# Attention with a token mix behind it: when GpSimd starts a pair's work, which output ScalarE drains first, and VectorE's order in the third step

## The chip, the cores and the metric

The kernel runs on one core of a Trainium2 chip. A core has five engines that run in parallel, each in its own program order: TensorE (PE in the profile; its weight loads are PEld), VectorE (DVE), ScalarE (ACT), GpSimd (POOL), and SyncE (SP), which issues the transfers. They wait for one another through counting semaphores. The metric is the device time of one execution in microseconds (us).

## The reference

Three layers in float32. The change touches the first and the hand-over to the second.

```python
# attention: 4 batches x 8 heads, 576 tokens, 64 channels per head
scores = 0.125 * q @ k.T
scores = where(scores >= max(scores) - tau, scores, -1e9)
attn = exp(scores - max(scores)); attn /= attn.sum() + 1e-9
x = attn @ v                                   # heads side by side: 576 x 512 per batch
# layer 2: token mix, then channel mix
u = x + (relu(x.T @ w_tok1) @ w_tok2).T         # 576 -> 256 -> 576 tokens
u = u + relu(u @ w_ch1) @ w_ch2                 # 512 -> 1536 -> 512
# layer 3: gated convolution over tokens
h = relu(u @ w_in); out = (h * sigmoid(conv3(h))) @ w_out
```

## The kernel before

**Units and steps.** Two heads make a pair; there are 16 pairs. The 576 queries of a pair are cut into five units: t = 0 to 3 hold 128 queries of both heads, t = 4 holds the last 64 queries of both. The function `bodies` calls a `body` on each engine for k = 0 to 18: k counts the pairs, and k = 16 to 18 only finish the last ones. `at.g` is the pair's number, `at.k` the same number as far as it is known when the program is built (k = 4 to 13 run in a hardware loop of two pairs, an even one and an odd one, for five turns). On PE, DVE and ACT a body has five steps s = 0 to 4.

**Softmax of a unit.** PE makes its scores (`scores`, L999, L1004). DVE copies them negated out of PSUM and takes the maximum (`copy_out`, L841). ACT makes exponentials and threshold (`exp_unit`, L591, L594). DVE masks (`mask`, L858): it reads the negated scores and the exponentials, both in SBUF, and writes `prob`. PE turns `prob` (L1025, L1034; the 64 columns that are left over are turned by L1064 and L1079 and called tails), and ACT drains what was turned into `probT` (`drain_turned_probs`, L608, L615, L617) and `probTt` (L624, L625, L631). In step s of pair g PE makes the scores of unit s+2 and turns those of unit s, and DVE copies unit s+2 and masks unit s+1, where s+2 and s+1 run over into the next pair.

**The output of a pair.** The product of pair g-1 with its values (PV) is made in steps 0 and 1 of body g: `times_v` (L1094), then `times_v_tail` (L1102), which raises `pv_done`. In step 2 ACT drains it to `oT` (L641 to L644), PE turns it (L1120, and L1112 in step 3), and the rows are scaled into `x32`: the last 64 queries by ACT in step 2 (`normalise_short`, L662, raises `short_x`), the other 512 by DVE in step 3 (`normalise`, L881, raises `x_done`). PE turns `x32` back in step 4 (`turn_back`, L1125, raises `xt_done`), and ACT drains that into `uy` (`drain_x`, L667, raises `xt_drained`).

There is one `x32`. Both who write it wait until the pair before has been split by GpSimd; `pair` is g-1 here, and `x_split` counts the pairs that are split:

```python
# ScalarE, normalise_short(pair, k), step 2
act.wait_ge(xa_tail_done, pair + 1)
act.wait_ge(inv_done, pair + 1)
if k >= 1:
    act.wait_ge(x_split, pair)
# VectorE, normalise(pair, k), step 3
if k >= 1:
    dve.wait_ge(x_split, pair)
```

TensorE's tail in step 3 (`turn_tails(at, 3)`, L1079 into `mixed`) waits for `short_x` of the same step.

**GpSimd's work.** Products in the mixes take each operand as a rounded part and a rest. GpSimd makes these: `split_x` (xh, L440, then the rest xl, L471), `rest_of_token` (h1l, L490, twice for two pairs together), the weights (`split_wt`, `split_weight`, `split_w1`), and `add_u` adds a pair's token mix to `uy` (L498). PE makes the token mix for two pairs at a time: in odd bodies `mix_hidden` (L1146, steps 3 and 4; waits for `x_split`), in even bodies `mix_out` (L1175: half a pair's output in step 2, the other half in step 3, and the next pair's in step 4; the first piece waits for `tok_lo`, which `rest_of_token` raises). ACT drains these in `drain_hidden` (L650, L651) and `drain_u` (L673). The first tails of each pair (`turn_first_tails`, L1064, end of step 0) go into the banks `mixed` and `out_t` and wait for these drains (`wait_for_banks`): for `hid_left` in even bodies, for `u_drained` in odd ones.

Of the kernel before, what the change touches and what calls it, by code (L numbers as in the profile page):

```python
# [22 lines left out]
P = 128  # L23

def build(nc, qk_in, v_in, tau, w_tok1, w_tok2, w_ch1, w_ch2, w_in, conv_w, w_out, out):
    PAIRS, _, S = qk_in.shape
# [16 lines left out]
    KM, KF, KC, KT = DM // P, DF // P, DC // P, DT // P  # L44
# [150 lines left out]
    with ctx:  # L195
# [38 lines left out]
        pv_done = sem("pv_done")  # L234
# [195 lines left out]
        def _(pool):  # L430
# [27 lines left out]
            xs_hi = sem("xs_hi")  # L458

            def split_x(at):  # L460
                pair = at.g - 1
                mine = slice((at.k - 1) % 2 * P, (at.k - 1) % 2 * P + P)
                pool.wait_ge(x_done, pair + 1)
                pool.wait_ge(short_x, pair + 1)
                if at.hid:
                    pool.wait_ge(tok_done, at.g - 1)
                pool.nop(nofuse=True)
                copy(xh[:, :, mine], x32[:, :, :]).then_inc(xs_hi, 1)
                pool.wait_ge(xs_hi, pair + 1)
                pool.nop(nofuse=True)  # L470
                nc.gpsimd.tensor_tensor(xl[:, :, mine], x32[:, :, :], xh[:, :, mine].bitcast(F32), ALU.subtract) \  # L471
                    .then_inc(x_split, 1)
# [12 lines left out]

            def rest_of_token(at, i):

                pool.wait_ge(hid_left, at.g - 2 + i)
                pool.nop(nofuse=True)
                nc.gpsimd.tensor_tensor(h1l[:, i, :], h1f[:, i, :], h1h[:, i, :].bitcast(F32), ALU.subtract) \  # L490
                    .then_inc(tok_lo, 1)
# [24 lines left out]

            def body(at):
                g, k = at.g, at.k
                if at.mix:
                    add_u(g - 4)  # L520
                for i in range(KT if at.hid else 0):
                    rest_of_token(at, i)
                if at.pv:
                    split_x(at)
                if at.mix:
                    add_u(g - 3)
                if k == 1:
                    split_wt(range(NT))
                if k == 2:
                    for kt in range(KT):  # L530
                        split_weight(wt2h[:, kt, :], wt2l[:, kt, :], wt2f[:, kt, :], wt_split)
                if k % 2 == 1 and k < 2 * W1_EARLY:
                    split_w1(g // 2, k == 1)

            bodies(pool, body)

            for c in range(W1_EARLY, KC):
                split_w1(c, False)
# [38 lines left out]
        def _(act):  # L577
# [124 lines left out]
            def body(at):  # L702
                g, k = at.g, at.k
                for s in range(NT):
                    if s == 0 and k == PAIRS:
                        round_first_u(0)
                        round_first_u(1)
                    if s == 2 and at.pv:
                        drain_out(g - 1, k - 1)
                    if s == 2 and at.units:  # L710
                        drain_first_tails(at)
                    if at.units:
                        drain_turned_probs(at, s)
                    if s == 4 and at.pv:
                        act.wait_ge(xt_done, g)
                        if not at.units:
                            drain_x_tail(g - 1)
                        drain_x(g - 1)
                    ahead = at.unit(s + 2)
                    if ahead:  # L720
                        exp_unit(ahead)
                    if s == 2:
                        if at.mix:
                            drain_u(g - 4, 0, 0)
                        if at.pv:
                            normalise_short(g - 1, k - 1)
                        if at.units:
                            drain_tail(at, 2)
                        if k == PAIRS + 1:
                            unit(0, 2, 3)  # L730
                    if s == 3:
                        if at.hid:
                            drain_hidden(at, 0)
                        if at.mix:
                            drain_u(g - 4, 1, 1)
                        if at.units:
                            drain_tail(at, 3)
                        if PAIRS <= k < PAIRS + 2:
                            unit(0, 3 * (k - PAIRS), 3 * (k - PAIRS) + 1)
                    if s == 4:  # L740
                        if at.hid:
                            drain_hidden(at, 1)
                        if at.mix:
                            drain_u(g - 3, 0, 1)
                            drain_u(g - 3, 1, 0)
                        if k == PAIRS:
                            unit(0, 1, 2)
# [74 lines left out]
        def _(dve):  # L822
# [76 lines left out]
            def body(at):  # L899
                for s in range(NT):  # L900
                    two, one = at.unit(s + 2), at.unit(s + 1)
                    if two:
                        copy_out(two)
                    if s == 4 and at.units:
                        invert_sums(at)
                    if one:
                        mask(one)
                    if s == 1 and at.k == PAIRS:
                        split_first_u()
# [463 lines left out]
```

## Time and profile before

| | |
|---|---|
| median of 3 runs | 849.05 us (848.79 to 851.71) |
| the profiled execution's own time | 850.66 us |
| its span in the trace | 848.9 us |
| busy share of the span: PE, PEld, DVE, ACT, POOL | 97%, 79%, 50%, 49%, 31% |
| granted TensorE clock, mean | 0.997 of full speed |
| chain of work that ended last: PE, DVE, ACT, issue | 84%, 6%, 6%, 3% |

The span is the time from the first to the last instruction of the trace; some 1.8 us of the execution lie around it. The shares are means over the three layers. The pairs fill the first 320 us or so, layer 2's channel mix the time to about 643 us, the third layer the rest. From k = 4 on the pairs repeat every 40.1 us for an even and an odd one together. A mean over the span says little of that stage, so the rows below are of two pairs in the middle of it, the even pair from about 168 us and the odd one from about 188 us.

### The profile page before, as it was taken

How to read it: one execution, taken by the hardware profiler on the slowest of the kernel's cores; microseconds unless marked ns; L12 is line 12 of the kernel's file. 1: busy time of each engine (PE TensorE's matmuls, PEld its weight loads, DVE VectorE, ACT ScalarE, POOL GpSimd, SP SyncE). 2: the span in 40 equal slices, each digit the busy share in tenths (PEclk: the TensorE clock that was granted, in tenths of full speed). 3: DMA queues.
4: the chain of work that ended last, by engine and by line, in shares of the span. 5: the costliest groups of instructions: out<-in, count | busy, mean ns of one | idle time of the engine just before them, and what ended most of it. 6: DMA issues, size and time to landing. Idle time of an engine off the chain costs nothing.

```text
span 848.9 us, 15131 instructions
## 1 busy us (share of the span) xinstructions
PE 824.3 (97%) x5656; PEld 669.5 (79%) x5656; DVE 422.5 (50%) x829; ACT 412.5 (49%) x914; POOL 265.7 (31%) x202
## 2 busy tenths in 40 slices
PE   8999999999999998899999999999999999999998
PEld 4666776767777766788888888888899989898996
DVE  6897878787877774501211211211214819156380
ACT  4887887877878785211211201211114737355461
POOL 0062415142332323470200100120291726428170
PEclk9999999999999999999999999999999999999999
DMA  9311111111111114000000000000320010100101
GB/s 266 111 48 47 48 48 46 46 46 46 46 46 46 50 16 149 1 1 0 1 1 1 0 1 1 1 0 1 128 71 2 1 51 1 45 17 0 49 0 62
DMA packets 20906, 32.70 MB, mean 39 GB/s; under 512 B 4416, under 2 KB 11136, under 8 KB 20864
## 3 DMA queue, kind: packets, MB, share of 16 engines
q1 hardware_dynamic: 20864, 32.13, 11.7%
q8 instruction: 28, 0.46, 0.2%
q14 instruction: 14, 0.11, 0.0%
HBM read 27.41 MB, written 4.72 MB: 38 GB/s over the span
## 4 chain that ended last, share of the span: by engine, by line
PE 84%; DVE 6%; ACT 6%; issue 3%; POOL 0%; ACTq 0%; DVEq 0%; POOLq 0%
PE score L1203 17%; PE score L1318 12%; PE score L999 5%; PE out_t L1218 4%; PE turn_y L1218 4%; PE mixed L1218 4%; PE turn_x L1218 4%; DVE prob L858 4%; PE out_t L1303 4%; PE out_t L1094 4%; PE mixed L1146 3%; PE mixed L1094 3%; PE turn_y L1303 3%; PE mixed L1303 3%; PE turn_x L1303 3%
## 5 line engine op out<-in xcount | busy, mean ns | idle before, releaser
L921 DVE SCALAR_TENSOR_TENSOR h<-score,h 128x512 fp32r<-128x512 f32 (+1 forms) x60 | 38.3, 638 | 243.5 <-ACT h L693 243.5
L693 ACT ACTIVATE h<-score 128x512 fp32r<-128x512 f32 (+1 forms) x60 | 33.3, 555 | 250.5 <-PE score L1203 250.5
L841 DVE TENSOR_SCALAR_CACHE_REDUCE negs<-score,neg_scale 128x576 f32<-128x576 f32 x144 | 112.7, 816 | 58.7 <-PE score L999 34.0
L858 DVE SCALAR_TENSOR_TENSOR prob<-negs,thresh,exps 128x576 f32<-128x576 f32 x144 | 134.2, 964 | 0.3 <-ACT thresh L594 0.3
L591 ACT ACTIVATE exps<-negs,neg_max 128x576 f32<-128x576 f32 x144 | 104.6, 772 | 1.9 <-DVE negs L841 1.5
L999 PE MATMUL score<-qk 64*128 64x288 f32 x512 | 85.5, 434 | 1.6 <-DVE negs L841 1.0
L1203 PE MATMUL score<-uh,w1h 128*128 128x512 f32 (+1 forms) x240 | 86.9, 368 | 0.0
L1203 PE MATMUL score<-uh,w1l 128*128 128x512 f32 (+1 forms) x240 | 86.8, 368 | 0.0
L1203 PE MATMUL score<-ul,w1h 128*128 128x512 f32 (+1 forms) x240 | 86.8, 368 | 0.0
L559 POOL TENSOR_TENSOR zl<-z,zh 128x512 fp32r<-128x512 f32 x32 | 54.2, 1694 | 98.7 <-ACT zh_t L779 98.7
L999 PEld LDWEIGHTS score<-qk 64*128 64x128 f32 x512 | 46.9, 188 | 28.0 <-issue 13.1
L506 POOL TENSOR_TENSOR ul<-uy,uh 128x256 fp32r<-128x256 f32 (+6 forms) x7 | 16.7, 2402 | 161.7 <-ACT uh L680 161.7
L961 DVE SCALAR_TENSOR_TENSOR conv<-hpad,cw,conv 128x576 f32<-128x576 f32 x32 | 27.2, 850 | 77.4 <-ACT conv L792 77.3
L1025 PEld LDWEIGHTS turn_x<-ident,prob 64*128 64x128 f32 x512 | 41.4, 139 | 22.1 <-issue 16.4
L608 ACT ACTIVATE probT<-turn_x 128x512 f32<-128x512 f32 x64 | 38.2, 596 | 41.0 <-PE turn_y L1025 40.3
L1318 PE MATMUL score<-yl,wih 128*128 128x288 f32 x256 | 54.9, 296 | 0.0
L1318 PE MATMUL score<-yh,wil 128*128 128x288 f32 x256 | 54.8, 296 | 0.0
L1318 PE MATMUL score<-yh,wih 128*128 128x288 f32 x256 | 54.8, 296 | 0.0
L1025 PE MATMUL turn_x<-ident,prob 64*128 64x64 f32 x512 | 46.8, 225 | 6.4 <-DVE prob L858 4.3
L490 POOL TENSOR_TENSOR h1l<-h1f,h1h 128x256 fp32r<-128x256 f32 x16 | 11.7, 728 | 127.7 <-ACT h1f L651 127.7
L1203 PEld LDWEIGHTS score<-uh,w1l 128*128 128x128 f32 x240 | 45.3, 189 | 7.6
L1203 PEld LDWEIGHTS score<-ul,w1h 128*128 128x128 f32 x240 | 45.3, 189 | 7.6
(184 smaller groups left out, 2010.0 us busy)
## 6 DMA issues: line engine op xcount, KB each, us to landing
qk<-in_qk SPq DMA_DIRECT2D x16, 640.0 KB, 3.9
vm<-in_v SPq DMA_DIRECT2D x16, 320.0 KB, 4.2
result<-ostage SPq DMA_DIRECT2D x16, 256.0 KB, 2.1
w1f<-in_moe_w_ch SPq DMA_DIRECT2D x4, 768.0 KB, 10.8
w2f<-in_moe_w_ch SPq DMA_DIRECT2D x4, 768.0 KB, 7.4
wif<-in_moe_w_in SPq DMA_DIRECT2D x1, 2048.0 KB, 7.8
wof<-in_moe_w_out SPq DMA_DIRECT2D x8, 256.0 KB, 2.6
wt2f<-in_moe_w_tok SPq DMA_DIRECT2D x1, 576.0 KB, 9.4
```

The source lines that it names most:

```text
L559: nc.gpsimd.tensor_tensor(zl[:, t, :], z32[:, t % 2, 0:MAIN], zh[:, t, :].bitcast(F32), ALU.subtract)
L591: nc.scalar.activation(exps[i][:, h, :], negs[:, i, h, :], ACT.Exp, bias=neg_max[:, i, h:h + 1], scale=-1.0).then_inc(exp_done, 1)
L841: nc.vector.tensor_scalar(negs[:, i, h, :].rearrange("p (c s) -> p c s", c=2), raw_of[h], neg_scale[:, 0:1], None, ALU.mult, ALU.min, accu ...
L858: nc.vector.scalar_tensor_tensor(out=prob[:, i, h * S:(h + 1) * S], in0=negs[:, i, h, :], scalar=thresh[:, i, h:h + 1], in1=exps[i][:, h, ...
L921: nc.vector.scalar_tensor_tensor(out=h3[:, n % RING, 1, 0:w], in0=hidden_banks[n % 4][:, 0:w], scalar=0.0, in1=h3[:, n % RING, 0, 0:w].bit ...
L999: mm = nc.tensor.matmul(score[:, 2 * h + c, 0:HALF], qT[par][rows, t * P:(t + 1) * P], kT[par][rows, halves[c]])
L1025: mm = nc.tensor.transpose(turn[r][:, to:to + D], prob[rows, i, k_at:k_at + P], ident[rows, rows])
L1094: nc.tensor.matmul(bank[mine, 0:HALF], vm[par][:, kt, mine], probT[par][:, h, kt, c * HALF:(c + 1) * HALF], start=(kt == 0), stop=False, s ...
L1203: mm = nc.tensor.matmul(hidden_banks[n % 4][:, 0:w], wt[:, c, kt, :], x[:, kt, 0:w], start=(i == 0), stop=(i == 3 * KM - 1))
L1218: mm = nc.tensor.matmul(sum_banks[mt][:, 0:w], wt[:, c, o:o + P], h3[:, n % RING, part, 0:w], start=(c == 0 and i == 0), stop=(c == KC - 1 ...
L1303: mm = nc.tensor.matmul(bank, z, wt[:, kt, :], start=(kt == 0 and n == 0), stop=(kt == KF - 1 and n == 2))
L1318: mm = nc.tensor.matmul(in_banks[c % 2][:, i, 0:HALF], wt[:, kt, c * P:(c + 1) * P], y[:, kt, i * HALF:(i + 1) * HALF], start=(n == 0), st ...
```

## The change

Three edits. On GpSimd each body that has a PV waits for it first. The parts of its work move by a body: the split of a pair's `x32` and the rest of the hidden tokens are made one body later than before, and the two `add_u` stand elsewhere. On ScalarE the drain of the output turned back (`drain_x`) stands ahead of the drain of the turned probabilities in step 4. On VectorE the mask of unit 3 stands ahead of the copy of unit 4 in step 2, the third step.

```diff
             def split_x(at):
-                pair = at.g - 1
-                mine = slice((at.k - 1) % 2 * P, (at.k - 1) % 2 * P + P)
+                pair = at.g - 2
+                mine = slice(at.k % 2 * P, at.k % 2 * P + P)
                 pool.wait_ge(x_done, pair + 1)
                 pool.wait_ge(short_x, pair + 1)
-                if at.hid:
-                    pool.wait_ge(tok_done, at.g - 1)
+                if at.mix:
+                    pool.wait_ge(tok_done, at.g - 2)
+                if 5 <= at.k and at.k % 2 == 1:
+                    pool.wait_ge(tok_done, at.g - 3)
                 pool.nop(nofuse=True)
...
             def rest_of_token(at, i):
 
-                pool.wait_ge(hid_left, at.g - 2 + i)
+                pool.wait_ge(hid_left, at.g - 3 + i)
...
             def body(at):
                 g, k = at.g, at.k
-                if at.mix:
+                if at.pv:
+                    pool.wait_ge(pv_done, g)
+                for i in range(KT if at.mix else 0):
+                    rest_of_token(at, i)
+                if k >= 5 and k % 2 == 1:
                     add_u(g - 4)
-                for i in range(KT if at.hid else 0):
-                    rest_of_token(at, i)
-                if at.pv:
+                if 2 <= k < PAIRS + 2:
                     split_x(at)
-                if at.mix:
-                    add_u(g - 3)
...
                 if k % 2 == 1 and k < 2 * W1_EARLY:
                     split_w1(g // 2, k == 1)
+                if at.mix:
+                    add_u(g - 4)
 
             bodies(pool, body)
+            add_u(PAIRS - 1)
...
                     if s == 2 and at.units:
                         drain_first_tails(at)
-                    if at.units:
-                        drain_turned_probs(at, s)
                     if s == 4 and at.pv:
                         act.wait_ge(xt_done, g)
                         if not at.units:
                             drain_x_tail(g - 1)
                         drain_x(g - 1)
+                    if at.units:
+                        drain_turned_probs(at, s)
...
             def body(at):
                 for s in range(NT):
                     two, one = at.unit(s + 2), at.unit(s + 1)
+                    if one and s == 2:
+                        mask(one)
                     if two:
                         copy_out(two)
                     if s == 4 and at.units:
                         invert_sums(at)
-                    if one:
+                    if one and s != 2:
                         mask(one)
```

**GpSimd, one turn of the hardware loop.** This is the even body and then the odd one, before. In the names x is `x32`, h1l and h1f are the hidden tokens' rest and value.

```order
L498 TENSOR_TENSOR uy<-u_part,uy 128x576
L440 TENSOR_SCALAR xh<-x_81 128x5x128 [waits x_done,short_x]
L471 TENSOR_TENSOR xl<-x_81,xh 128x5x128 [waits xs_hi]
...
L498 TENSOR_TENSOR uy<-u_part,uy 128x576
...
L490 TENSOR_TENSOR h1l<-h1f,h1h 128x256 [waits hid_left] x2
...
L440 TENSOR_SCALAR xh<-x_81 128x5x128 [waits tok_done,x_done,short_x]
L471 TENSOR_TENSOR xl<-x_81,xh 128x5x128 [waits xs_hi]
...
L447 TENSOR_TENSOR w1h<-w1f,ones 128x512
...
L483 TENSOR_TENSOR w1l<-w1f,w1h 128x512 [waits chunk_hi]
```

And the same turn of the changed kernel:

```order
L490 REGISTER_ALU [waits pv_done]
L492 TENSOR_TENSOR h1l<-h1f,h1h 128x256 [waits hid_left]
...
L492 TENSOR_TENSOR h1l<-h1f,h1h 128x256 [waits hid_left]
...
L440 TENSOR_SCALAR xh<-x_81 128x5x128 [waits tok_done,x_done,short_x]
L473 TENSOR_TENSOR xl<-x_81,xh 128x5x128 [waits xs_hi]
...
L500 TENSOR_TENSOR uy<-u_part,uy 128x576
...
L496 ISA [waits pv_done]
...
L500 TENSOR_TENSOR uy<-u_part,uy 128x576
L440 TENSOR_SCALAR xh<-x_81 128x5x128 [waits tok_done,x_done,short_x]
L473 TENSOR_TENSOR xl<-x_81,xh 128x5x128 [waits xs_hi]
```

The even body now begins behind `pv_done` with both h1l, then xh and xl, then one addition; the odd body behind its `pv_done` with an addition, then xh and xl, then the weights as before. The xh and xl of an even body belonged to the pair whose PV that body finished; now they belong to the pair ahead of it.

**VectorE, steps 1 to 3 of an even pair in the loop.** L841 is a copy, L858 a mask, L881 `normalise`. Before:

```order
L858 SCALAR_TENSOR_TENSOR prob,rowsum<-negs,thresh,exps_71 128x576
...
L858 SCALAR_TENSOR_TENSOR prob,rowsum<-negs,thresh,exps_71 128x576
...
L841 TENSOR_SCALAR negs,neg_max<-score,neg_scale 128x576
...
L858 SCALAR_TENSOR_TENSOR prob,rowsum<-negs,thresh,exps_79 128x576
...
L858 SCALAR_TENSOR_TENSOR prob,rowsum<-negs,thresh,exps_79 128x576
...
L841 TENSOR_SCALAR negs,neg_max<-score,neg_scale 128x576 x2
```

And of the changed kernel:

```order
L863 SCALAR_TENSOR_TENSOR prob,rowsum<-negs,thresh,exps_71 128x576
...
L863 SCALAR_TENSOR_TENSOR prob,rowsum<-negs,thresh,exps_71 128x576
...
L863 SCALAR_TENSOR_TENSOR prob,rowsum<-negs,thresh,exps_79 128x576
...
L863 SCALAR_TENSOR_TENSOR prob,rowsum<-negs,thresh,exps_79 128x576
...
L846 TENSOR_SCALAR negs,neg_max<-score,neg_scale 128x576
...
L846 TENSOR_SCALAR negs,neg_max<-score,neg_scale 128x576 x2
```

The two masks of unit 3 (exps_79) now follow straight on those of unit 2, and the single copy of unit 4 comes behind them.

**ScalarE, step 4 of an even pair in the loop**, before:

```order
L631 ACTIVATE probTt_72<-mixed 128x128
...
L599 ACTIVATE uy<-turn_x 128x64
L615 ACTIVATE probT_74<-turn_x 128x4x64
L617 ACTIVATE probTt_72<-turn_x 64x64
L615 ACTIVATE probT_74<-turn_y 128x4x64
L617 ACTIVATE probTt_72<-turn_y 64x64
...
L667 ACTIVATE uy<-out_t 128x512
...
L591 ACTIVATE exps_71<-negs,neg_max 128x576
```

And of the changed kernel:

```order
L636 ACTIVATE probTt_72<-mixed 128x128
...
L672 ACTIVATE uy<-out_t 128x512
...
L604 ACTIVATE uy<-turn_x 128x64
L620 ACTIVATE probT_74<-turn_x 128x4x64
L622 ACTIVATE probTt_72<-turn_x 64x64
L620 ACTIVATE probT_74<-turn_y 128x4x64
L622 ACTIVATE probTt_72<-turn_y 64x64
...
L596 ACTIVATE exps_71<-negs,neg_max 128x576
```

The drain of `out_t` into uy has moved from behind the five drains to ahead of them.

## Rows read from the trace of the kernel before

**Rows 1.** Busy time of each engine in the 20 us of an even pair

```profile
core 0: us, PE busy (x) PEld busy (x) DVE busy (x) ACT busy (x) POOL busy (x), PEclk, DMA share, GB/s
180.00:200.00 20.00, 19.16 (x187) 13.66 (x184) 16.48 (x42) 16.64 (x43) 5.84 (x4) 1.00 0.18 58
```

**Rows 2.** Who waited for whom, two pairs (168.08 to 208.16): total, times, longest

```profile
PE out_t L1175 <- ACT uy L667: 0.5, 1, 0.5
PEld mixed L1079 <- ACT x L662: 0.4, 1, 0.4
PE turn_x L1025 <- DVE prob L858: 0.4, 1, 0.4
```

**Rows 3.** Timeline of ACT: start, length, [idle before]; even pair, then odd

```profile
179.44 0.63 ACT L662 ACTIVATE x<-mixed,rinv 64x64 f32<-64x64 f32 x2
...
184.67 0.60 ACT L667 ACTIVATE uy<-out_t 128x512 f32 x1
...
186.98 0.40 ACT L673 ACTIVATE u_part<-out_t 128x288 f32<-128x288 f32 x1
...
198.70 0.63 ACT L662 ACTIVATE x<-mixed,rinv 64x64 f32<-64x64 f32 x2
...
203.82 0.22 ACT L599 ACTIVATE uy<-turn_x 128x64 f32 x1 [0.81 <-PE turn_y L1042]
...
207.21 0.38 ACT L651 ACTIVATE h1f<-mixed 128x256 f32<-128x256 f32 x1
```

**Rows 4.** Timeline of PE in the same two pairs

```profile
174.92 0.65 PE L1102 MATMUL mixed<-probTt,vm 128*128 128x288 f32 x2
...
183.34 0.66 PE L1125 MATMUL out_t<-ident,x 128*128 128x128 f32 x4
...
187.88 0.22 PE L1064 MATMUL mixed<-ident,prob 64*128 64x64 f32 x1
...
194.47 0.65 PE L1102 MATMUL mixed<-probTt,vm 128*128 128x288 f32 x2
...
203.59 0.65 PE L1125 MATMUL out_t<-ident,x 128*128 128x128 f32 x4
...
207.74 0.24 PE L1064 MATMUL mixed<-ident,prob 64*128 64x64 f32 x1
```

**Rows 5.** Timeline of POOL around the even pair

```profile
167.64 0.73 POOL L490 TENSOR_TENSOR h1l<-h1f,h1h 128x256 fp32r<-128x256 f32 x1 [4.04 <-ACT h1f L651]
168.34 0.72 POOL L440 TENSOR_SCALAR xh<-x 128x640 fp32r<-128x640 f32 x1
169.21 1.86 POOL L471 TENSOR_TENSOR xl<-x,xh 128x640 fp32r<-128x640 f32 x1
...
188.23 1.40 POOL L498 TENSOR_TENSOR uy<-u_part,uy 128x576 f32 x1
```

**Rows 6.** Timeline of POOL in the third pair, no mask beside it

```profile
62.29 1.54 POOL L471 TENSOR_TENSOR xl<-x,xh 128x640 fp32r<-128x640 f32 x1
```

**Rows 7.** Timeline of DVE: masks and copies from the even pair on

```profile
168.64 1.03 DVE L858 SCALAR_TENSOR_TENSOR prob<-negs,thresh,exps 128x576 f32<-128x576 f32 x1
...
169.60 2.09 DVE L858 SCALAR_TENSOR_TENSOR prob<-negs,thresh,exps 128x576 f32<-128x576 f32 x1
...
176.69 0.82 DVE L841 TENSOR_SCALAR_CACHE_REDUCE negs<-score,neg_scale 128x576 f32<-128x576 f32 x1 [1.30 <-PE score L1004]
...
177.43 0.82 DVE L858 SCALAR_TENSOR_TENSOR prob<-negs,thresh,exps 128x576 f32<-128x576 f32 x1
...
188.34 0.81 DVE L841 TENSOR_SCALAR_CACHE_REDUCE negs<-score,neg_scale 128x576 f32<-128x576 f32 x1
```

**Rows 8.** Timeline of the last pair's body: PE, then ACT

```profile
330.85 0.65 PE L1102 MATMUL mixed<-probTt,vm 128*128 128x288 f32 x2
...
333.88 0.62 ACT L662 ACTIVATE x<-mixed,rinv 64x64 f32<-64x64 f32 x2
```

**Rows 9.** Timeline of the last pair's body: DVE

```profile
331.54 2.36 DVE L891 TENSOR_TENSOR ul<-uy,uh 128x1024 fp32r<-128x1024 f32 x2 [9.91 <-PE mixed L1102]
```

## The prediction

> **What bounds the kernel now.** I first looked at the busy time of the engines in a stretch of 20 us in the pairs [rows 1]: PE is busy for 19.16 us, DVE for 16.48, ACT for 16.64, POOL for 5.84, at full clock. So PE sets the pace, and a change matters where PE waits or comes to wait. The waits of two pairs [rows 2] name where it stops: 0.5 us for ACT's drain into uy (L667), 0.4 us for a mask of DVE (L858), and 0.4 us of its weight loads for ACT's x (L662, `normalise_short`). Those are small, so PE is nearly gapless; but they tell which chain runs level with it. The timelines of ACT and PE [rows 3, 4] show that chain: PV ends on PE, ACT makes x, PE's tail of step 3 goes on from x, turns back, ACT drains uy and then u_part or h1f, and PE's first tails (L1064) of the next pair follow. The even x ends at 179.44 + 0.63 = 180.07, the odd one at 198.70 + 0.63 = 199.33. I call these ends X. Whatever moves X moves PE, since neither engine has more than some 0.4 us to give behind it.
>
> **The change part by part. GpSimd.** The code says that x of pair g-1 may be written only when pair g-2 is split (`x_split`). Before, that split was made in the body before, long ahead. Now it is made in the same body, and only after `pv_done` of this body. So a new chain stands between PV's end and X: GpSimd's whole work up to xl.
>
> Even body. PV ends at 174.92 + 0.65 = 175.57 [rows 4]. A fulfilled wait and the start behind it take about 0.15 (L1064 at 207.74 behind h1f, which ends at 207.21 + 0.38 = 207.59) [rows 3, 4]; with two waits ahead of the first h1l I take 0.2. Then 0.73 + 0.73 for h1l, 0.72 for xh, 0.15 between xh and xl, and 1.54 for xl [rows 5, 6]: 3.87 us, which ends at 179.64 if nothing holds it. ACT used to start x at 179.44. Into this stretch VectorE's edit puts both masks of unit 3, which before began at 177.43 and now can begin as soon as PE's tail behind PV is turned, at about 175.8. Taking turns they hold GpSimd twice for 0.6 (0.82 less what overlaps): 1.2 us. So `x_split` comes at 180.85, ACT starts 0.1 later, and X is 181.6 instead of 180.07: +1.5. Without any holding it would be 179.64 + 0.1 + 0.63 = 180.37: +0.3. These are the two bounds; I take the upper one since the masks are ready within 0.1 us of GpSimd's first instruction.
>
> What else waits in the even body: PE's first `mix_out` piece for both h1l (0.2 + 0.73 + 0.6 + 0.73 = 2.3 us after PV's end with one mask between), and the scores of step 3 for the copy of unit 4, which moves from 176.69 to about 178.4. Both cost PE 0.5 to 1 us by themselves, but PE then has to wait for X anyway; they are in the 1.5, not on top.
>
> Odd body. PV ends at 194.47 + 0.65 = 195.12 [rows 4]. Ahead of xh stands one addition of 1.40 with three more waits (0.35 to its start): 0.35 + 1.40 + 0.72 + 0.15 + 1.54 = 4.16, so 199.28, and with the two masks 200.45. X is 201.2 instead of 199.33: +1.85; unheld 200.0: +0.7. Here even the unheld work is late, since ACT started x at 198.70.
>
> Queued behind the waiting x on ACT are a tail, the probabilities of step 3 and the next exponentials; on PE the tail of step 3 and all behind it. The transfers are not moved: the loads of V wait for `pv_done` as before.
>
> **ScalarE.** In step 4 ACT now waits first for the output turned back. In the even pair that ends at 183.34 + 0.66 = 184.0 [rows 4], while ACT's five drains of this step began at 183.56 before and now begin 0.6 later behind the drain into uy. The work is the same, its start is 0.5 later, and so are the exponentials and u_part behind it: u_part ended at 186.98 + 0.40 = 187.38 [rows 3], now 187.9, and L1064, which ran at 187.88 [rows 4], needs it: +0.2. The 0.5 that PE waited for uy [rows 2] is gone, but PE spends it at L1064. In the odd pair ACT began at 203.82 after an idle 0.81, and now waits for 203.59 + 0.65 = 204.24: 0.5 later, and h1f, which L1064 follows within 0.15, is 0.5 later too: +0.5. I take these; the bounds are 0 and 0.2 for the even pair, 0.4 and 0.6 for the odd one.
>
> **What it frees.** With GpSimd through by step 4, masks of steps 0 and 1 are no longer stretched. PE loses its wait of 0.4 for a mask [rows 2]: −0.4 for each two pairs. The other stretched masks have nobody waiting.
>
> **The holding and the skill.** The row shows a mask at 168.64 issued 0.30 us after an xh of 0.72, thus with 0.42 of it left, and lengthened by only 1.03 − 0.82 = 0.21 [rows 5, 7]. I therefore took some 0.2 off each holding. The Trainium skill, "SBUF — State Buffer", section "Who interferes with whom", says that whoever issues first holds the shared port pair for the whole instruction and the other blocks fully, for a VectorE instruction with two SBUF inputs against a GpSimd one that reads SBUF. By the rule in full each of the four holdings would cost 0.2 more and the sum below 5 us more, about 882.
>
> **The sum.** Two pairs: 1.5 + 0.2 + 1.85 + 0.5 − 0.4 = 3.65 us. The pairs k = 4 to 15 are six such twos: 21.9. For k = 0 to 3 there is no h1l and no addition; GpSimd needs 0.35 + 0.72 + 0.15 + 1.54 = 2.8 and 4.0 with masks, close to when x is wanted (3.87 behind PV, going by the even pair), and the late copy and ScalarE's edit remain: I estimate 1.5 in all, from 0 to 3. For the last pair GpSimd starts behind 330.85 + 0.65 = 331.50 with 0.2 + 3.87, and beside it lies DVE's L891, 2.36 us with two inputs in SBUF [rows 8, 9]; `x_split` falls between 335.6 and 337.9, where ACT made x at 333.88: 1.8 to 4, I take 3. And in k = 17 the addition of 1.40 now stands ahead of the last split (2.4), which `mix_hidden` waits for: another 2, from 0 to 4. Together 5. The total is 21.9 + 1.5 + 5 = 28.4. The profiled execution took 850.66 (its span of 848.9 and 1.8 around it), so 879.1; that execution lies 1.6 above the median of 849.05, so **877**.
>
> **The rivals.**
> - *GpSimd is not held by the masks* (they go through as a pair, or GpSimd as a whole). Then two pairs cost 0.3 + 0.2 + 0.7 + 0.5 − 0.4 = 1.3, six of them 7.8, and with 0.5 and 3 for the ends 849 + 11 = 860. For it speaks only that the order of issue is within 0.1 us; against it the mask of 2.09.
> - *Faster*: GpSimd's work is through before x is wanted, and what counts is that masks are free of it and uy is drained first. The place is `x_split` against ACT's L662; it decides where GpSimd is done by 179.4 and 198.7. Gain 0.4 + 0.5 a two, 5.4 in all: 844. Against it stands that the plain sum of its instructions, 3.87 and 4.16 with starts, is longer than the 3.87 and 3.58 between PV's end and x.
> - *No change*: PE takes the delays up elsewhere, 849. Against it: PE is busy 19.16 of 20, so it can't catch up 3.65 in 40.
> - *Worse than forecast*: the new waits on POOL cost more each, and the late copy and late h1l add to X. With 4.8 a two, 29 and 3 and 8 for the ends: 889.
>
> **How the numbers follow.** Chances: forecast (868 to 886) 0.68, not held 0.19, worse 0.05, faster 0.04, no change 0.04. The range leaves out the last three and the lower side of "not held": 860 to 886. A measurement of this kernel tells 0.5% from no change, about 4 us; by the cases faster 0.04, within 0.5% 0.04, slower 0.92.
>
> **What would show it.** In the changed profile: two pairs repeat every 43.7 us instead of 40.1. ACT's x (L662's successor) waits for POOL xl, 1.5 us and more, in every pair from k = 4; it starts some 5.3 us behind PV's end. In step 2 the masks of unit 3 and POOL's first instructions are stretched, and the masks of steps 0 and 1 last 0.82. L1064 waits for u_part and h1f. The prediction is wrong if ACT's x waits for nobody, or if two pairs take under 41 us; if x waits but for less than 0.5 us, the holding was mis-sized.

## The result, and the profile after

| | before | changed |
|---|---|---|
| median (lowest to highest) | 849.72 us (848.79 to 851.71) | 884.60 us (883.77 to 885.91) |
| profiled execution, its span | 850.66, 848.9 | 885.37, 883.6 |
| mean granted clock of TensorE | 0.997 | 0.984 |
| two pairs, from L1064 of k = 4 to k = 14, a fifth | 40.11 us | 43.78 us |

The changed kernel is slower: ratio 1.041, interval 1.038 to 1.043. That is 34.7 us of span. Line numbers of the changed kernel are up to 7 higher than before: L440 stays, L662 is L667, L858 is L863, L1064 is L1071.

The page of the changed kernel, busy times, granted clock in 40 slices, and the chain that ended last by engine:

```profile
PE 833.2 (94%) x5656; PEld 677.3 (77%) x5656; DVE 421.5 (48%) x829; ACT 415.6 (47%) x914; POOL 265.8 (30%) x202
...
PEclk9988999999999999899999999999999999999999
...
PE 81%; ACT 5%; issue 5%; POOL 4%; DVE 4%; DMA 1%; ACTq 0%; POOLq 0%; SPq 0%; DVEq 0%
```

POOL has the same work as before and was on 0% of the chain then; now it holds 4% of it. Its busy time tells nothing of this: 30% of the span.

The waits of two pairs of the changed kernel (204.73 to 248.16): total, times, longest, answering to [rows 2]:

```profile
PE score L1006 <- DVE negs L846: 2.0, 2, 1.6
ACT exps L596 <- DVE negs L846: 1.6, 2, 0.9
PE mixed L1086 <- ACT x L667: 1.1, 2, 0.6
ACT x L667 <- POOL xl L473: 1.0, 2, 0.7
...
PE mixed L1071 <- ACT h1f L656: 0.6, 1, 0.6
PE mixed L1071 <- ACT u_part L678: 0.6, 1, 0.6
```

PE's waits for uy and for a mask of [rows 2] are gone. PE now waits for x, for h1f and u_part, and, longest of all, for a copy (`negs`) ahead of the scores of step 3.

The changed kernel's timeline of POOL, odd pair, then even pair, then the last, answering to [rows 5]:

```profile
212.56 1.83 POOL L500 TENSOR_TENSOR uy<-u_part,uy 128x576 f32 x1 [10.93 <-PE mixed L1109]
214.36 1.23 POOL L440 TENSOR_SCALAR xh<-x 128x640 fp32r<-128x640 f32 x1
215.75 1.55 POOL L473 TENSOR_TENSOR xl<-x,xh 128x640 fp32r<-128x640 f32 x1 [0.15 <-POOL xh L440]
...
234.58 1.93 POOL L492 TENSOR_TENSOR h1l<-h1f,h1h 128x256 fp32r<-128x256 f32 x2 [14.86 <-PE mixed L1109]
236.48 1.23 POOL L440 TENSOR_SCALAR xh<-x 128x640 fp32r<-128x640 f32 x1
237.85 1.54 POOL L473 TENSOR_TENSOR xl<-x,xh 128x640 fp32r<-128x640 f32 x1
...
361.03 3.33 POOL L492 TENSOR_TENSOR h1l<-h1f,h1h 128x256 fp32r<-128x256 f32 x2 [13.03 <-PE mixed L1109]
```

POOL stands idle for 10.9 us in the odd pair and 14.9 us in the even one. It starts 0.49 and 0.23 us behind the end of PV, and ACT's x waits for its xl. The timeline of DVE in the even pair beside it:

```profile
232.86 0.82 DVE L863 SCALAR_TENSOR_TENSOR prob<-negs,thresh,exps 128x576 f32<-128x576 f32 x1
...
234.58 1.34 DVE L863 SCALAR_TENSOR_TENSOR prob<-negs,thresh,exps 128x576 f32<-128x576 f32 x1 [0.90 <-PE out_t L1086]
...
235.85 1.27 DVE L863 SCALAR_TENSOR_TENSOR prob<-negs,thresh,exps 128x576 f32<-128x576 f32 x1
...
237.05 0.81 DVE L846 TENSOR_SCALAR_CACHE_REDUCE negs<-score,neg_scale 128x576 f32<-128x576 f32 x1
```

The mask of unit 2 at 232.86, with POOL idle, lasts 0.82. Both masks of unit 3 start with POOL's work and take 1.34 and 1.27 (in the odd pair, where the first starts ahead of the addition, 0.82 and 1.96). The copy for which PE's scores of step 3 wait stands behind them. ACT and PE of the changed kernel, x and what hangs on it, answering to [rows 3, 4]:

```profile
217.41 0.64 ACT L667 ACTIVATE x<-mixed,rinv 64x64 f32<-64x64 f32 x2 [0.65 <-POOL xl L473]
...
239.51 0.64 ACT L667 ACTIVATE x<-mixed,rinv 64x64 f32<-64x64 f32 x2 [0.35 <-POOL xl L473]
```

```profile
211.42 0.65 PE L1109 MATMUL mixed<-probTt,vm 128*128 128x288 f32 x2
...
233.70 0.65 PE L1109 MATMUL mixed<-probTt,vm 128*128 128x288 f32 x2
...
240.20 0.33 PE L1086 MATMUL mixed<-ident,prob 128*128 128x128 f32 x1 [0.54 <-ACT x L667]
...
248.16 0.24 PE L1071 MATMUL mixed<-ident,prob 64*128 64x64 f32 x1 [0.60 <-ACT u_part L678]
```

The even x ends at 240.15, 5.80 us behind the end of PV (234.35); the odd one at 218.05, 5.98 behind 212.07. In [rows 3, 4] these were 4.50 and 4.21.

### The profile page after: what moved, and what is told of

Its sections match the earlier page's. It is cut to its first block, busy times and chain, and to the rows that moved or that the text cites. A ratio compares the mean times of both kernels' runs of the same rounds, so it can differ in the third digit from the quotient of the medians.

```text
span 883.6 us, 15155 instructions
## 1 busy us (share of the span) xinstructions
PE 833.2 (94%) x5656; PEld 677.3 (77%) x5656; DVE 421.5 (48%) x829; ACT 415.6 (47%) x914; POOL 265.8 (30%) x202
## 4 chain that ended last, share of the span: by engine, by line
PE 81%; ACT 5%; issue 5%; POOL 4%; DVE 4%; DMA 1%; ACTq 0%; POOLq 0%; SPq 0%; DVEq 0%
PE score L1210 17%; PE score L1325 12%; PE score L1006 6%; PE out_t L1101 4%; PE out_t L1225 4%; PE turn_y L1225 4%; PE mixed L1225 4%; PE turn_x L1225 4%; PE out_t L1310 4%; PE mixed L1101 4%; PE turn_y L1310 2%; PE mixed L1310 2%; PE turn_x L1310 2%; DVE prob L863 2%; PE mixed L1153 2%
## 5 line engine op out<-in xcount | busy, mean ns | idle before, releaser
L863 DVE SCALAR_TENSOR_TENSOR prob<-negs,thresh,exps 128x576 f32<-128x576 f32 x144 | 134.3, 965 | 13.9 <-PE out_t L1086 12.5
L1006 PE MATMUL score<-qk 64*128 64x288 f32 x512 | 88.0, 444 | 18.6 <-DVE negs L846 18.4
L500 POOL TENSOR_TENSOR uy<-u_part,uy 128x576 f32 (+1 forms) x16 | 26.3, 1643 | 101.6 <-PE mixed L1109 65.7
L1210 PEld LDWEIGHTS score<-uh,w1h 128*128 128x128 f32 x240 | 45.7, 191 | 7.5
```

The source lines that it names most:

```text
L863: nc.vector.scalar_tensor_tensor(out=prob[:, i, h * S:(h + 1) * S], in0=negs[:, i, h, :], scalar=thresh[:, i, h:h + 1], in1=exps[i][:, h, ...
L1006: mm = nc.tensor.matmul(score[:, 2 * h + c, 0:HALF], qT[par][rows, t * P:(t + 1) * P], kT[par][rows, halves[c]])
L1210: mm = nc.tensor.matmul(hidden_banks[n % 4][:, 0:w], wt[:, c, kt, :], x[:, kt, 0:w], start=(i == 0), stop=(i == 3 * KM - 1))
```

## The experiments

All times are medians; "two pairs" is the measure of the table above. A dip is a fall of TensorE's granted clock to half. Where two lengths are given without dips, they are those of an even and an odd body in the loop whose clock stayed full. Bodies, X and dips are read from the one profiled execution of each kernel.

**1. GpSimd's edit alone.** The orders of ScalarE and VectorE are those of before.

> GpSimd's edit alone, the orders of ScalarE and VectorE as before. Theory 1 (the split of the pair before, made only after PV, holds up ScalarE's x): most of the loss is here, 18 to 26 us above before, and ScalarE's x waits for GpSimd's xl in every pair of the loop. The masks of unit 3 then stand behind the copy of unit 4, so that copy is on time and TensorE's scores of step 3 don't wait. Theory 2 (the loss is VectorE's late copy of unit 4 behind masks that GpSimd holds): under 8 us above before.

Measured: 873.28 us (868.14 to 874.49), ratio 1.027 (1.025 to 1.030). Two pairs 42.32, bodies without a dip 20.42 + 21.15. X comes 5.10 and 5.33 behind PV. The waits of two pairs of this kernel (151.8 to 193.37):

```profile
PE turn_x L1030 <- DVE prob L863: 2.4, 2, 1.6
...
ACT x L667 <- POOL xl L473: 1.5, 2, 1.0
...
PE out_t L1180 <- ACT uy L672: 0.5, 1, 0.5
```

23 of the 34.7 us are here, with the same wait of x for POOL. But another wait is larger: PE stands before it turns the probabilities of unit 3, for a mask that POOL holds up.

**2. ScalarE's edit alone, and the change without it.**

```
+ if s == 4 and at.pv:
+     ...
+     drain_x(g - 1)
  if at.units:
      drain_turned_probs(at, s)
```

> ScalarE's edit alone. The five drains of step 4 and all behind them start 0.5 us later, TensorE's first tails wait 0.2 us (even pair) and 0.5 us (odd pair) longer, and up to 0.4 us of that is taken up by the mask that TensorE waits for anyway: 0.3 to 0.7 us for two pairs, 2 to 5 us in all above before. If the drain into uy was what bound the even pair, it is a gain of up to 3 us instead.

Measured: 853.78 us, ratio 1.004 (1.003 to 1.006), 3.5 us; two pairs 40.38 (19.85 + 20.50, before 20.24 + 19.85). So the even body is 0.39 shorter, the odd one 0.65 longer. Of the 3.1 us by which the span grew, 0.4 stand in the first four pairs and 1.6 behind L1064 of k = 15.

> The whole change but ScalarE's edit. Alone it cost 3.5 us; within the change the first tails wait for the same drains, so it should cost 3 to 5 us there too, and this be 880 to 882 against 884.6. If it costs nothing beside the waits for GpSimd, this is 884 to 885.

Measured: 879.45 us, a little under what was expected, ratio 1.036 (1.034 to 1.037); two pairs 42.75, without dips 20.96 + 21.61; X at 5.80 and 5.96 as with the full change. So the edit costs 3.5 us alone and 5.2 on top of the others, and it does not move X: it is a cost behind x. In two pairs without dips it is 0.3 alone and 0.9 on top of the others (21.17 + 22.29 with it), so it is not the same cost in both.

**3. VectorE's edit alone, from the fifth pair alone, and the change without it.**

```
+ if one and s == 2:                      (alone)
+ if one and s == 2 and at.k >= 4:        (from the fifth pair)
+     mask(one)
  if two:
      copy_out(two)
  ...
```

> VectorE's edit alone; GpSimd is idle in step 2, so nothing holds the masks. The copy of unit 4 ends 0.5 us later. Theory 1: from -1 to +3 us against before, most of it in the first four pairs. Theory 2 (the order alone is what costs): 10 us or more above before.

Measured: 855.45 us, ratio 1.006 (1.005 to 1.008), 5.2 us where at most 3 were expected. Two pairs are 40.09, as before. L1064 of k = 4 comes at 90.88 instead of 87.47: 3.4 of the 5.2 arise in the first four pairs, whose bodies last 16.33, 18.63, 20.53 and 20.94 (before 14.62, 18.23, 18.51, 21.46). In the first of them POOL splits nothing yet; a mask ahead of a copy that PE is waiting for is enough. PE waits 6.0 us for `negs` between 10 and 90, in 7 times (before: 1.0 in 2).

> VectorE's edit alone and only from k = 4 on. The run with it in all pairs was 5.2 us above before, of which the trace shows 3.4 in the first four pairs and none in the loop. Theory: those pairs are paced by VectorE, and only there does the mask ahead of the copy cost; so this is within 1.5 us of before. If the edit costs through the clock or in the last pairs, it is 2 to 5 us above.

Measured: 849.62 us, ratio 1.000 (0.999 to 1.001). From k = 4 on the edit is free. Of the 5.2 us of the edit from the first pair on, all is thus owed to what it does in the first four. This run is a second look at the first four pairs of before as well, where the two kernels are the same: they took 71.70 us from L1064 of k = 0 to that of k = 4, without a dip, and 72.82 in before, whose fourth body had one (20.36 against 21.46).

> The whole change but VectorE's edit. Theory 1: 20 to 28 us above before, of the 35 of the whole change; the x of a pair still ends 5 us or more behind PV. The first four pairs lose 2 us or less instead of 8, since their loss is the copy of unit 4 behind held masks. Theory 2: less than 10 us above before.

Measured: 878.22 us, ratio 1.033 (1.030 to 1.035), 28.0 us, the top of what was expected; two pairs 43.51, X 5.10 and 5.33 behind PV. L1064 of k = 4 comes at 90.73, 3.3 later than before, where at most 2 were expected: GpSimd's and ScalarE's edits together also cost something there.

**4. Two buffers for x.** With `x32s[k % 2]`, pair k writes x once pair k-2 is split, which is long done. The wait of x for POOL goes, all else of the change stays.

```
+ x32s = [s1.put(f"x32_{i}", [P, NT, P]) for i in range(2)]
...
- if k >= 1:
-     act.wait_ge(x_split, pair)
+ if k >= 2:
+     act.wait_ge(x_split, pair - 1)
```

> The whole change with two x32 in turn, so that neither ScalarE's x nor VectorE's normalise waits for the split of the pair just ahead. The holding of the masks by GpSimd and the late copy of unit 4 stay. Theory 1 (split behind PV): x no longer waits for GpSimd, but now comes behind the late copy and its exponentials: its end goes from 5.8 and 6.0 us behind PV to some 5.4 in both kinds of pair. Two pairs take 42.3 to 42.8 us instead of 43.5, the whole 873 to 880. If the wait for the split was not what bound, the time stays within 2 us of 884.6.

Measured: 880.16 us (879.29 to 882.29), ratio 1.035 (1.033 to 1.037); two pairs 43.11, without dips 20.69 + 21.53. That is the upper end of the 873 to 880 expected; 42.3 to 42.8 had been expected for two pairs. Nobody waits for xl any more, and only 4.4 us come back. X still ends 5.34 and 5.20 behind PV, late behind the copy. The waits of two pairs (160.41 to 202.63):

```profile
PE score L1011 <- DVE negs L849: 1.9, 2, 1.6
```

The scores of step 3 wait for the copy of unit 4 just as in the full change. That wait was no by-product of x's lateness: it stands nearly level with it. The next run therefore also takes VectorE's order back.

> The change without VectorE's edit, and with two x32. Both gates are gone: the wait for the split and the late copy behind held masks. Theory 1: x ends 4.5 and 4.2 us behind PV as before, two pairs take 40.2 to 40.6 us (ScalarE's edit is left), the whole 852 to 859, of which up to 4 come from the last pair's h1l behind PV. If GpSimd costs in another way (its waits, its holding of masks elsewhere), it stays above 865.

Measured: 874.57 us (872.06 to 877.59), ratio 1.028 (1.024 to 1.031), and 852 to 859 had been expected: a clear miss. X was back at 4.51 and 4.21, as before the change, and still the bodies without a dip were 20.63 + 20.95. One of its waits in two pairs (197.8 to 241.74), and of its timelines a row of POOL and one of DVE at the same moment:

```profile
PE turn_x L1036 <- DVE prob L866: 2.4, 2, 1.6
```

```profile
230.95 1.86 POOL L474 TENSOR_TENSOR xl<-x,xh 128x640 fp32r<-128x640 f32 x1
...
231.34 2.09 DVE L866 SCALAR_TENSOR_TENSOR prob<-negs,thresh,exps 128x576 f32<-128x576 f32 x1
```

The mask of unit 3 stands behind xl for 1.27 us, and PE's turning of unit 3 waits for this mask. Both orders of VectorE lose: mask first makes the copy late, copy first makes the mask late.

> A version meant to beat both: GpSimd's edit and two x32, the orders of ScalarE and VectorE as before, no wait for PV in the last pair's body and there the last split ahead of the addition. GpSimd then works in step 2 and 3, where VectorE waits for scores anyway, and masks of steps 0 and 1 are free. Theory 1: TensorE's wait of 0.4 us for a mask in two pairs is gone and x is on time: two pairs 39.7 to 40.1 us, the whole 845 to 850. If the masks of unit 3 and 4 are held and delay x's tail instead, 850 to 856.

Here ScalarE's edit is out as well, GpSimd does not wait for PV in the last pair's body, and in k = 17 the split stands ahead of the addition. Measured: 864.27 us (861.72 to 866.61), ratio 1.015 (1.013 to 1.018), two pairs 42.05, X on time. 845 to 850 had been expected, or 850 to 856 by the rival: both missed. The same wait, in its waits of 173.92 to 215.46:

```profile
PE turn_x L1038 <- DVE prob L868: 2.4, 2, 1.6
```

Up to the last pairs this kernel differs from that of experiment 1 by the two buffers alone. X ends at 4.51 and 4.21 behind PV instead of 5.10 and 5.33, and two pairs without dips take 20.41 + 21.14 instead of 20.42 + 21.15. With VectorE's order of before, the late x thus costs nothing in the loop: PE waits for the mask.

**5. GpSimd does not wait for PV.** All else of the change stays, the order of GpSimd's work too.

```
- if at.pv:
-     pool.wait_ge(pv_done, g)
```

> The whole change without GpSimd's wait for PV; the parts stay one body later in its program, but each starts as soon as what it needs is there, which for a split is the end of the pair's x in the body before. Theory 1: x doesn't wait for GpSimd, masks of unit 3 are not held, two pairs take 40.2 to 40.6 us, and the whole is near the sum of the other two edits alone, 855 to 861. If it is the new order on GpSimd that costs and not the start behind PV, it stays above 870.

Measured: 859.86 us (859.24 to 861.54), ratio 1.011 (1.009 to 1.013); two pairs 40.67, X 4.51 and 4.49. One wait carries 24.7 of the 34.7 us. What is left, 9.5, is near the 3.5 and 5.2 of the other two edits, though not at the same places: 6.8 of it stand in the first four pairs. Its waits of two pairs (195.4 to 236.05) are those of ScalarE's and VectorE's edits:

```profile
PE mixed L1069 <- ACT u_part L676: 1.2, 2, 0.6
...
PE score L1004 <- DVE negs L844: 0.9, 1, 0.9
```

**6. The split behind the masks of unit 3.** The kernel of 864.27 with one more wait ahead of the split:

```
+ if 4 <= k and at.units:
+     pool.wait_ge(mask_done, TILES * g + 2 * FULL)
  if 2 <= k < PAIRS + 2:
      split_x(at)
```

> The kernel of the run before (two x32, GpSimd's edit, orders of ScalarE and VectorE as before), and in the bodies from k = 4 GpSimd splits only when both masks of unit 3 are done; before that it does only h1l or the addition, which end while VectorE still copies. There the split of 2.4 us lies beside copies of the next pair, which it can't hold. Theory 3 (what remained in the runs with two x32 is the masks of unit 3 held by the split, and TensorE's turning behind them): two pairs fall from 40.8 us (and 42.1 with the dips of the clock) to 39.7 to 40.2, the granted clock is back at 0.997, the whole is 846 to 852. If the remaining loss came from the start behind PV itself or from the waits on GpSimd, it stays above 858.

Measured: 859.25 us (858.83 to 859.87), ratio 1.011 (1.010 to 1.013); 846 to 852 had been expected. Half came true: PE no longer waits for a mask in the loop, and the even body is 19.65, shorter than before the change (20.24). The odd one is 20.96, and the waits of 191.04 to 231.66 say why:

```profile
PE mixed L1162 <- POOL xl L474: 0.9, 1, 0.9
```

Now the split is too late for its own reader, `mix_hidden`; waits on GpSimd were the rival that the expectation named. But this is the smaller part: of the 8.8 us by which the span exceeds that of before, 2.7 stand in the first four pairs, where the new wait does not apply, 2.2 in the loop and its next pair, and 3.9 behind k = 15. None of the places behind PV that were tried, for two subtractions, an addition and a split, leaves everybody undisturbed.

**7. A version that follows from this.** Kernel of before, with two buffers for x, and GpSimd's body in another order. From k = 4 each body waits for the masks of unit 3, and none for PV. Even bodies split two pairs, each split followed by an addition; odd bodies have no split, make the weights and take the h1l subtractions last. PE's, ACT's and DVE's orders are untouched.

```
+ if 4 <= k and at.units:
+     pool.wait_ge(mask_done, TILES * g + 2 * FULL)
+ if at.mix and k <= PAIRS:
+     split_x(at, 2)
  if at.mix:
      add_u(g - 4)
...
+ if at.pv and (k < 3 or at.mix):
+     split_x(at, 1)
...
+ for i in range(KT if at.hid else 0):
+     rest_of_token(at, i)
```

> The kernel before, meant to be beaten, with two x32 and GpSimd's work placed by what the runs showed: from k = 4 a body's work on GpSimd starts when both masks of unit 3 are done, both splits of two pairs are made in the even body, w1 in the odd one ahead of h1l. So no long GpSimd instruction lies beside the masks of steps 0, 1 and 2, and the odd pair's hidden products find both splits made. Theory 3 (only where GpSimd holds masks, and who waits for the split, counts): TensorE's wait of 0.4 us for a mask in two pairs is gone, two pairs take 39.4 to 39.8 us instead of 40.1, the whole is 845.5 to 849 against 850. If holding of unit 4's mask or of the next pair's takes its place, 850 to 853.

Measured: 846.15 us (845.46 to 848.16), ratio 0.996 (0.994 to 0.997); two pairs 39.53. Its waits of two pairs (185.94 to 225.46), and its POOL:

```profile
PE out_t L1186 <- ACT uy L673: 0.5, 1, 0.5
PE mixed L1089 <- ACT x L668: 0.2, 1, 0.2
```

```profile
216.94 0.73 POOL L440 TENSOR_SCALAR xh<-x 128x640 fp32r<-128x640 f32 x1 [10.41 <-DVE prob L865]
217.82 1.56 POOL L472 TENSOR_TENSOR xl<-x,xh 128x640 fp32r<-128x640 f32 x1
...
222.58 1.25 POOL L440 TENSOR_SCALAR xh<-x 128x640 fp32r<-128x640 f32 x1
```

The wait for a mask of [rows 2] is gone, the first split lies beside DVE's copies of step 3 (217.25 to 218.8) and lasts what it lasts alone [rows 6]. The second, at 222.58, still lies beside masks, and PE shows no wait for one. It beats both kernels, the one before by 0.4%: a small gain, but its six executions (845.46 to 848.16) all lie below the eleven of before beside them (848.80 to 850.75).

## Why the prediction came out

The time was forecast as 877 in 860 to 886, and it is 884.6. The chain that the prediction named, from PV over GpSimd to x, is there and has the length it gave. It is not the only gate, as the prediction took it to be, one term was far too small, and the clock, which had no term, brought some others near their mark.

**X, right.** The chain from PV through POOL to x was forecast 6.0 and 6.1 us long and measured 5.80 and 5.98; X moved by 1.30 and 1.77 where 1.5 and 1.85 stood in the sum. In the even pair the start took 0.23 (forecast 0.2), in the odd one 0.49 (0.35), and xl what it takes. The holding was 0.95 and 0.91 instead of 1.2: in the even pair two subtractions and xh, 2.18 us by [rows 5], ran from 234.58 to 237.71, which is 3.13; in the odd one an addition and xh, 2.12 us, ran from 212.56 to 215.59, which is 3.03. The Trainium skill, "SBUF — State Buffer", section "Who interferes with whom", has the two engines exclude each other fully; 2.18 and two masks of 0.82 would then be 3.82 one behind the other. The rows give 3.13: POOL's three and DVE's two alternate with four handovers, at each of which the spans lie side by side for 0.14 to 0.21 us. Two neighbours on one engine do so too, for 0.04 to 0.08 us, so some of this may be the way the spans are taken. The rule's direction holds, its size is above what is measured here, and the 882 that the prediction gave by it would have been nearer the result for a reason that is not the rule. One comparison in the prediction is off: against "faster" it sets 3.87 us of GpSimd's work against 3.87 between PV's end and x in the even pair and calls the first longer. With the start of 0.2 it is 4.07, so the argument stands.

**Two pairs, right, for a reason that was half of it.** 43.7 was forecast, 43.78 measured. Without dips it is 43.46 (21.17 even, 22.29 odd, against 20.24 and 19.85), which is 3.37 more where the sum had 3.65; that the dips brought it to 3.67 is luck. From k = 4 on the prediction's sum was 26.9 (21.9 and 5), and the span grew by 26.3 (34.7 less the 8.4 below). But it said that PE's waits for the late copy and the late h1l are "in the 1.5, not on top", as if x were the one gate. Experiment 4 shows gates of nearly equal height: with the wait of x for POOL gone, 4.4 us came back, where the sum gives 20 to X (1.5 and 1.85, six times); in two pairs without dips 1.24 came back of the 3.35. With x and VectorE's order restored, another 5.6 came back, and a third gate was left, the held masks, behind which a late x costs nothing. So the step "PE then has to wait for X anyway" holds only in the sense that the waits stand side by side; X alone was not worth 20 us. What moves all of them together is POOL's start behind PV: 24.7 us in experiment 5.

**The first four pairs, wrong.** The term was 1.5 us (0 to 3) and measured 8.4: L1071 of k = 4 comes at 95.88, L1064 came at 87.47. The step that failed is that without h1l and additions only "the late copy and ScalarE's edit remain", at 1.5 in all. The same row of the experiments, against before:

| kernel | L1064 of k = 4 | from L1064 of k = 0 | dips between |
|---|---|---|---|
| before itself | 87.47 | 72.82 | 1 |
| experiment 3, from the fifth pair: here as before | -1.9 | -1.1 | 0 |
| GpSimd alone | +0.2 | +1.0 | 0 |
| ScalarE alone | +0.4 | +0.5 | 1 |
| VectorE alone | +3.4 | +3.6 | 1 |
| GpSimd and ScalarE | +3.3 | +3.3 | 1 |
| GpSimd and VectorE | +6.3 | +7.0 | 3 |
| all, without the wait for PV | +6.8 | +6.8 | 2 |
| all | +8.4 | +9.1 | 4 |

The column from L1064 of k = 0 leaves out the start, which comes up to 0.85 us earlier or later in single executions of kernels that are the same up to there. One execution of before and one of a kernel that is the same in these pairs are 1.1 us apart by a single dip, so differences of 1 us say nothing here.

VectorE's edit is the largest part, 3.4 alone and 5.1 on top of GpSimd's and ScalarE's: here PE waits for copies, and a mask ahead of one is a delay in full. GpSimd's edit does not make x late here by itself (X stays 4.21 behind PV, as the prediction had it), but in experiment 1 PE waits 1.3 us for a mask in the second of the four bodies, where the longest such wait before was 0.4. But the edits don't add, and the clock is one reason, as the last column shows. GpSimd's edit alone and with ScalarE's give PE the same waits in the third pair (0.9 us for masks, 0.8 for `negs`), yet the body lasts 18.88 in the one and 20.57 in the other. The windows of that stretch, columns as in [rows 1], of GpSimd's edit alone:

```profile
48.00:67.00 19.00, 17.26 (x168) 11.67 (x170) 16.15 (x40) 15.02 (x37) 7.64 (x6) 1.00 0.14 53
```

and with ScalarE's, whose body is the one from 48.99 to 69.56:

```profile
48.00:67.00 19.00, 16.70 (x146) 10.79 (x146) 14.47 (x35) 12.77 (x31) 7.65 (x6) 0.91 0.15 53
```

A granted clock of 0.91 instead of 1.00 goes with 1.7 us. The changed kernel has such a fall in three of the four bodies, and twice in the third. Its timeline of PE in the third pair:

```profile
50.29 1.22 PE L1101 MATMUL out_t<-probT,vm 128*64 128x288 f32 x4
...
55.73 0.71 PE L1101 MATMUL out_t<-probT,vm 128*64 128x288 f32 x4
...
63.48 0.87 PE L1006 MATMUL score<-qk 64*128 64x288 f32 x4 [2.33 <-DVE negs L846]
```

and its windows of 20 us:

```profile
20.00:40.00 20.00, 17.31 (x160) 12.14 (x159) 15.49 (x43) 14.07 (x34) 0.37 (x1) 0.91 0.32 88
40.00:60.00 20.00, 18.04 (x146) 11.59 (x145) 15.05 (x36) 14.63 (x36) 9.23 (x13) 0.91 0.16 50
60.00:80.00 20.00, 17.43 (x160) 12.16 (x160) 15.77 (x40) 14.63 (x36) 6.65 (x6) 0.91 0.15 50
80.00:100.00 20.00, 17.16 (x171) 13.62 (x171) 13.49 (x32) 13.58 (x36) 5.15 (x4) 0.91 0.15 51
```

The granted clock is 0.91 in each of the four; before, it was 1.00, 1.00, 0.91 and 1.00. Four PV matmuls at 50.29 take 1.22 us, at 55.73 the same take 0.71. The prediction had no term for the clock: it priced a wait of PE by its length alone.

**ScalarE, right in kind.** Forecast 0.2 and 0.5 in two pairs, 4.2 in six; measured 3.5 alone and 5.2 on top of the others. The near total is partly luck: alone, two pairs cost 0.27, the even body is even 0.39 shorter, and 1.6 us stand behind k = 15, for which there was no such term. L1071 waits for h1f and u_part as said.

**The last pair and k = 17, right in sum by luck.** Forecast 5, plus some 2 for k = 15; from L1071 of k = 15 to the end of the span 6.9 were added. From the end of the last PV to the end of the last `mix_hidden` it is 26.65 us instead of 21.32, which is 5.3. But k = 17 has next to no part in it: with the same order of GpSimd there, experiment 5 needs 21.39, and in the changed kernel PE waits for no xl there; the 2 us were not there. The last pair, at 3 in the sum, cost all of it. X moved as forecast, from 3.00 to 6.65 behind PV (1.8 to 4 had been said), but PE waited first for another thing: the two h1l subtractions took 3.33 us where 1.46 is their plain time, beside DVE's `ul`, which is L891 of [rows 9], and PE waited 2.31 for them. There the clock fell too, which had no term; the window, columns as in [rows 1]:

```profile
360.00:372.00 12.00, 8.27 (x30) 6.54 (x29) 6.20 (x5) 2.28 (x7) 7.59 (x5) 0.72 0.00 1
```

**The signs given.** ACT's x waits for POOL, but for 0.35 and 0.65 us, not 1.5 and more: since the scores of step 3 are late, ACT comes to x later too. The prediction would read a wait under 0.5 as a mis-sized holding; it was mis-sized, but by 0.25 to 0.3 us only, and the rest of the missing wait is ACT's own lateness. Its start is 5.16 and 5.34 behind PV's end, as forecast (5.3). The masks of steps 4, 0 and 1 last 0.76 to 0.82 from 223.67 to 233.68, as forecast; one of the odd pair's later steps (218.58, 1.76) lies beside POOL's weight work, which follows the split. None of the rivals came; "worse" named the late copy, but had it add to X in the loop, where two pairs stayed at 3.67 and not 4.8 above before. It added in the first four pairs.

**What stays open.** How much of the 34.7 is clock is only estimated. Executions of one kernel differ with the mean granted clock: before, 848.73 at 0.999 and 851.49 at 0.995; experiment 1, 868.14 at 0.992 and 874.44 at 0.984. That is about 0.8 us for each 0.001, and 0.997 to 0.984 would be some 10 us. It is no separate part beside the terms above, since the dips lie in them, and no run held the clock while it kept the waits. Why the edits don't add in the first four pairs was followed only in the one body above. No run repeats the profile of one kernel, so how often a body has a dip is not known.

## What to carry to other kernels

An engine with much idle time is not free to start when it likes: its instructions and another engine's can hold one another up, as here POOL's and the masks, and what counts is what that other engine does then and who waits for it. Look for every consumer of a late chain, not only the first; where several waits stand nearly level, removing one returns little: 4.4 of 34.7 us here. And read the first pairs by themselves: an order that is free in the steady loop cost 5 us in the first four.

## What was not expected of the hardware

A queued POOL instruction gets in between two masks of DVE that stand one behind the other, and the reverse, so in the rows looked at each side was delayed by one instruction of the other at a time, not by the whole group. With the masks at 1.34 and 1.27, the two engines took 2.54 and 3.13 us for 1.64 and 2.18 of work. The prediction read this from one place of before; it held in the pairs looked at of the changed kernel and of experiments 4 and 7.

Waits of PE of 0.7 to 2.3 us were followed by a fall of the granted clock from its full 2.4 GHz to 1.2 GHz in some bodies and not in others: a wait of 0.72 in the fourth body of before was, the same wait in the same body of experiment 3 (from the fifth pair) was not. A body with such a fall lasts 0.7 to 2.4 us more than its neighbours: the odd bodies of the changed kernel 22.3, and 23.00 or 23.13; those of experiment 1 21.15, and 22.62 or 23.27; the odd ones with two buffers and VectorE's old order 20.95, and 23.3. This also goes with the spread: the four times of experiment 1 lie within 6.4 us.
